# Reading the last five slots of a spilled transform back in halves: one FNet-style mixer with two feed-forward layers on one Trainium2 core

## The reference

```python
X = rfft(x, axis=1)
Yr = Xr @ w_r - Xi @ w_i + b_r
Yi = Xr @ w_i + Xi @ w_r + b_i
Y = soft_threshold(Yr, 0.01) + 1j * soft_threshold(Yi, 0.01)
y = irfft(Y, n=3008, axis=1)
# then on the 6016 tokens of y
h = y @ w_in;  y = (h * cos(h)) @ w_out          # 256 -> 2048 -> 256
h = y @ w_in2; y = (h * relu6(h + 3) / 6) @ w_out2
```

## Time and profile before

| | us |
|---|---|
| median of 3 runs | 1222.8 (1222.67 to 1222.94) |
| the profiled execution's own time | 1223.17 |
| its span, first to last instruction | 1221.4 |
| TensorE busy in it | 1201.1 (98%) |
| granted TensorE clock, mean | 0.994 of full speed |

### The profile page before, as it was taken

How to read it: one execution, slowest core, us unless ns; L and a number is a source line. 1 busy time by engine, 2 the same in 40 slices (tenths; PEclk the granted TensorE clock), 3 DMA queues, 4 the chain that set the end, 5 groups by cost and what they waited for, 6 DMA issues and landing times.

```text
span 1221.4 us, 14607 instructions
## 1 busy us (share of the span) xinstructions
PE 1201.1 (98%) x5576; PEld 1009.9 (83%) x5576; DVE 606.0 (50%) x599; ACT 631.1 (52%) x705; POOL 560.0 (46%) x294
## 2 busy tenths in 40 slices
PE   8999979899999999999999999999999999999998
PEld 8888779798888888888888888888888888888887
DVE  2787727655435445445454344444354354354344
ACT  2677646665545545445444445545455454454443
POOL 2577656774444433444334444344444444434410
PEclk9999989999999999999999999999999999999999
DMA  9488523000000100100001001001001001000000
GB/s 245 144 246 230 143 101 137 18 1 1 31 1 1 35 1 0 34 0 15 19 0 34 0 0 34 0 0 34 0 0 34 0 0 34 0 1 18 1 18 18
DMA packets 26149, 49.76 MB, mean 41 GB/s; under 512 B 3155, under 2 KB 9939, under 8 KB 25979
## 3 DMA queue, kind: packets, MB, share of 16 engines
q1 hardware_dynamic: 26114, 49.29, 13.4%
HBM read 31.06 MB, written 18.32 MB: 40 GB/s over the span
## 4 chain that ended last, share of the span: by engine, by line
PE 95%; DMA 2%; DVE 2%; ACT 1%; SPq 0%; issue 0%; POOL 0%; DVEq 0%; ACTq 0%
PE banks L586 41%; PE banks L636 41%; PE banks L491 2%; PE banks L511 2%; PE banks L506 2%; PE banks L507 2%; PE banks L564 2%; PE banks L526 1%; PE banks L527 1%; DMA v<-y_spill 1%; DMA y_spill<-y 1%; DMA xb<-in_x 0%; PE banks L542 0%; PE banks L540 0%; PE banks L539 0%; DVE phase L988 0%
## 5 line engine op out<-in xcount | busy, mean ns | idle before, releaser
L1167 POOL TENSOR_TENSOR gal<-ga,gah 128x1024 fp32r<-128x1024 f32 (+1 forms) x93 | 221.6, 2383 | 515.4 <-ACT gah L819 515.4
L984 DVE SCALAR_TENSOR_TENSOR phase<-phase,banks 128x1024 f32<-128x1024 int32 (+1 forms) x96 | 114.9, 1197 | 273.5 <-ACT phase L803 273.5
L1173 POOL TENSOR_TENSOR gbl<-gb,gbh 128x1024 fp32r<-128x1024 f32 (+1 forms) x88 | 206.6, 2348 | 16.6 <-ACT gbh L863 16.6
L811 ACT ACTIVATE cosine<-phase,half_pi 128x1024 f32<-128x1024 f32 (+1 forms) x96 | 109.1, 1136 | 192.8 <-DVE phase L988 192.1
L803 ACT ACTIVATE phase<-banks 128x1024 int32<-128x1024 f32 (+1 forms) x96 | 97.0, 1011 | 155.5 <-PE banks L586 154.9
L1006 DVE TENSOR_TENSOR ga<-banks,cosine 128x1024 f32<-128x1024 f32 (+1 forms) x96 | 115.4, 1203 | 104.8 <-ACT cosine L811 97.2
L1059 DVE SCALAR_TENSOR_TENSOR gb<-ramp,banks 128x1024 f32<-128x1024 f32 (+1 forms) x95 | 113.8, 1198 | 101.8 <-ACT ramp L848 101.8
L848 ACT ACTIVATE ramp<-banks,three 128x1024 f32<-128x1024 f32 (+1 forms) x95 | 104.3, 1098 | 108.9 <-PE banks L586 108.9
L863 ACT ACTIVATE gbh<-gb 128x1024 fp32r<-128x1024 f32 (+1 forms) x95 | 99.2, 1044 | 35.9 <-DVE gb L1059 31.6
L586 PE MATMUL banks<-xl,w1h 128*128 128x512 f32 (+1 forms) x384 | 116.8, 386 | 0.0
L586 PE MATMUL banks<-xh,w_lo 128*128 128x512 f32 (+1 forms) x384 | 116.7, 385 | 0.0
(11 more groups left out here) (107 smaller groups left out, 1853.1 us busy)
## 6 DMA issues: line engine op xcount, KB each, us to landing
w<-in_w_ff SPq DMA_DIRECT2D x32, 256.0 KB, 6.1
xb<-in_x SPq DMA_DIRECT2D x32, 192.0 KB, 6.7
y_spill<-y SPq DMA_DIRECT2D x24, 256.0 KB, 2.5
xf<-x_spill SPq DMA_DIRECT2D x11, 512.0 KB, 4.4
v<-y_spill SPq DMA_DIRECT2D x7, 780.0 KB, 7.1
x_spill<-xs SPq DMA_DIRECT2D x11, 470.0 KB, 3.2
out_y<-yt SPq DMA_DIRECT2D x10, 512.0 KB, 3.4
dbs<-in_db SPq DMA_DIRECT2D x24, 128.0 KB, 3.1
```

What stands on the lines that cost most here:

```text
L811: act.activation(cosine[:, :, 0:w], phase[:, :, 0:w], ACT.Sin, bias=half_pi[:, :], scale=-1.0).then_inc(a_cos, 1)
L984: dve.scalar_tensor_tensor(out=phase[:, :, 0:w], in0=phase[:, :, 0:w].bitcast(i32), scalar=-2.0 * math.pi, in1=bank[:, at:at + 2, 0:w], op ...
L1167: pool.tensor_tensor(gal[p % 2][:, :, 0:w], ga[:, :, 0:w], gah[p % 2][:, :, 0:w].bitcast(fp32), ALU.subtract).then_inc(a_gl, 1)
L1173: pool.tensor_tensor(gbl[pb % 2][:, :, 0:w], gb[:, :, 0:w], gbh[pb % 2][:, :, 0:w].bitcast(fp32), ALU.subtract).then_inc(b_gl, 1)
```

## The change

On SyncE, the seventh read of three whole slots (18 to 20) becomes three reads: the sine blocks (15 rows of 26 KB) at the old place, the cosine blocks (15 rows of 24 KB) later, and the cosine remainder (15 rows of 2 KB) behind write 23. Slots 21 and 22 are no longer read slot by slot in their sine blocks but together, as ten rows of 26 KB, after both are written. Their cosine remainder moves behind the read of slot 23 and is read with that slot's, 15 rows. The two remainder reads have a semaphore of their own, `v_rest_in`, which TensorE waits for before `cosine_part(12)`; before `cosine_part(0)` it now waits for three reads instead of four. The bytes read are the same.

```diff
-        v_idle_in = sem("v_idle_in")
+        v_idle_in, v_rest_in = sem("v_idle_in"), sem("v_rest_in")
...
             written(LAST_K - 3)
-            read_v(LAST_K - 2 - BATCHED, BATCHED, 0, BLOCKS, v_in)
+            read_v(LAST_K - 5, 3, FULL, FULL + 1, v_sin_in)
             for i in range(LAST_K - 2, LAST_K):
                 write_v(i)
             for i in range(LAST_K - 2, LAST_K):
                 written(i)
-                read_v(i, 1, FULL, FULL + 1, v_sin_in)
+            read_v(LAST_K - 2, 2, FULL, FULL + 1, v_sin_in)
+            read_v(LAST_K - 5, 3, 0, FULL, v_cos_in)
             read_v(LAST_K - 2, 2, 0, FULL, v_cos_in)
             write_v(LAST_K)
-            read_v(LAST_K - 2, 2, BLOCKS - 1, 1, v_cos_in)
+            read_v(LAST_K - 5, 3, BLOCKS - 1, 1, v_rest_in)
             written(LAST_K)
             read_v(LAST_K, 1, 0, FULL, v_cos_in)
-            read_v(LAST_K, 1, BLOCKS - 1, 1, v_cos_in)
+            read_v(LAST_K - 2, 3, BLOCKS - 1, 1, v_rest_in)
...
-            pe.wait_ge(v_in, 16 * (LAST_K - 2) // BATCHED)
+            pe.wait_ge(v_in, 16 * (LAST_K - 5) // BATCHED)
             pe.wait_ge(v_sin_in, 2 * 16)
             pe.wait_ge(v_idle_in, 16)
...
-            pe.wait_ge(v_cos_in, 4 * 16)
+            pe.wait_ge(v_cos_in, 3 * 16)
             for g in range(GROUPS):
+                if g == FULL:
+                    pe.wait_ge(v_rest_in, 2 * 16)
                 cosine_part(g)
```

## The result

The changed kernel takes 1220.24 us in the median of 16 runs (1219.63 to 1221.35), the kernel before 1222.84 (1222.22 to 1223.72): 2.60 us less, ratio 0.9979 with a 95% interval of 0.9971 to 0.9987. The forecast was 1220.0. The profiled execution has 1220.21 us with a span of 1218.4, so 1.8 us lie around the span, as before. The kernel before was run again beside each set of experiments; its median moved between 1222.47 and 1223.50 us from set to set, so medians of different sets are compared only through it.

A forecast was written before the change was run, and what follows sets the result against it. The prediction took TensorE's waits of 5.98 us at sine(0) and 0.50 us at cosine_part(0) as what could be gained. Its terms, 2.61 + 0.2 = 2.8 us, gave 1220.0 us, with a range of 1219.2 to 1221.8.

The forecast's parts named there:

- What bounds the kernel: TensorE's two waits on reads of v: 5.98 us at sine(0), 0.50 us at cosine_part(0); everything later hangs on TensorE.
- Part 1: Writes before sine(0): write 22 lands 1.99 us after issue, so SyncE's next issue comes 1.22 us earlier.
- Part 2: Joined sine read of slots 21 and 22 lands in 4.58 us; sine(0) 2.61 us earlier together with Part 1.
- Part 3: idft2(23)'s wait for y_lo from GpSimd: ready at 156.02, needed near 158.8, covered by 2.8 us.
- Part 4: Moved cosine reads ahead of write 23: engines clear by 158.1, write issued at 159.9, covered by 1.8 us, no cost.
- Part 5: cosine_part(0) no longer waits for the 10 KB remainder read: gain 0.2 us, between nothing and 0.50.
- The sum: Whole kernel: 2.61 + 0.2 = 2.8 us gained, from 1222.8 to 1220.0 us.
- over 0.2%: Whole kernel's median: faster by more than 0.2%, 2.45 us, so below 1220.35 us; chance 0.60.
- Rival B: Transfers before sine(0) hold each other up: write 22 takes 2.5 us, sine packets reach 5.3 us; 1221.4; chance 0.16.
- Rival C: TensorE's clock returns no earlier in the run, so sine matmuls end last before cosine_part(0); 1221.1 us; chance 0.07.
- Rival D: Queued reads share the engines instead of standing in line: sine(0) at 159.1, 1223.2 us; chance 0.07.
- Rival E: The change does not reach the end because something later has its own clock: 1222.8 us; chance 0.04.

The follow-up runs named there:

- e3: Kernel before, with only the cosine remainders on their own semaphore, waited for before cosine_part(12); 1222.73 us, ratio to before 0.9999.
- e1: Kernel before, with only the sine reads of slots 21 and 22 joined into one of ten rows; 1222.27 us, ratio to before 0.9992.
- e2: Kernel before, with only the read of slots 18 to 20 split into halves, sine reads of 21 and 22 separate; 1221.76 us, ratio 0.9988.
- e11: Changed kernel, with the joined sine read of slots 21 and 22 undone into two reads; 1220.86 us, ratio to before 0.9988.
- e6: Changed kernel, with both remainder reads waited for before cosine_part(0) again; 1220.38 us, ratio to before 0.9975.
- e7: Changed kernel, with the joined sine read cut: the seven blocks needed first, then the other six; 1218.64 us, ratio to before 0.9960.
- e4: Changed kernel, with the cosine read of slots 18 to 20 issued ahead of the joined sine read; 1221.99 us, ratio to before 0.9993.
- e5: Changed kernel, with unread matmuls added in TensorE's pauses around dft2(23), 6 ahead and 16 behind; 1223.00 us, ratio to before 0.9995.
- e9: Changed kernel, with unread matmuls added around dft2(23): 6 of 512 columns ahead, 32 of 256 behind; 1219.90 us, ratio to before 0.9976.
- e12: The same kernel as e9, run once more; 1219.24 us, ratio to before 0.9974.

## Why the prediction was right, and where its parts were not

**What bounds the kernel.** Right: two waits, 5.98 and 0.50 us, and nothing later took the gain back. The stretch from cosine_part(0) to the end is 1052.4 and 1052.3 us.

**Part 1, the freed writes.** Right: write 22 in 2.00 us (1.99 forecast). From write 21's issue to the first sine read 3.08 us instead of 4.25, 1.17 less (1.22 forecast).

**Part 2, the joined read.** Its landing was well priced (4.70 us, 4.58 forecast), and so was sine(0): 2.44 us nearer to write 21, 2.61 forecast. But of the "2.61 us for parts 1 and 2" part 1 had 1.22, which leaves 1.39 for the joining, and that split is wrong. sine(0) after write 21, in us, with two traces where there are two:

| | sine reads slot by slot | joined |
|---|---|---|
| slots 18 to 20 whole | 10.46, 10.02 (before, e3) | 9.88 (e1) |
| slots 18 to 20 in halves | 8.65, 8.47 (e2, e11) | 8.02, 8.17 (changed, e6) |

By the means the split is worth 1.7 to 1.8 us either way and the joining 0.4 to 0.5; both together 2.1 by these pairs, 2.44 by the first two traces alone. Four fifths of the gain are the first edit's. The pieces say why. Before, slot 22's read leaves 5.00 us after write 21: write 21 takes 4.23, and then SyncE spends 0.71 on slot 21's read first. In e11 it leaves after 3.02, as slot 21's read went out a microsecond before, so the split alone takes away SyncE's 0.7 us too, which the prediction had given to the joining. The read then takes 5.21 us to land in both, and the joining, which leaves at 3.08, only cuts that to 4.70. Why it is still 5.21 in e11, where its packets hardly wait for slot 21's, stays open. The sum came out right because it was taken along the chain and not as two gains; that it came within 0.2 us is in part luck, since single traces differ by 0.4.

**Part 3**, y_lo: covered, as said; sine(0) was followed by idft2 without a pause. **Part 4**: right, the engines were clear by 158.3 (158.1 forecast), write 23 left at 159.85 (159.9) and landed in 1.99 us.

**Part 5**, the remainders: 0.2 us forecast; 4.16 us from issue to landing against 4.39. e3 and e6 bound it between nothing and 0.3. In the four traces that wait for the remainders (before, e1, e2, e6) the data are there 3.9 to 4.4 us after the read's issue, in the changed kernel, e3, e11 and e7, which do not, after 3.8 to 4.3. The term is too small to be shown here, and nothing is as good a price as 0.2.

**The sum.** 2.8 us forecast; 2.67 to cosine_part(0) and 2.60 in the median. It lies beyond the 2.45 us of the 0.2% bound, but the interval (0.9971 to 0.9987) reaches past 0.998, so the "over 0.2%" that had 0.60 is not proved.

**Rival B**, slower transfers: no; 2.00 and 4.70 us. **Rival C**, the clock: this was closer than its 0.07. The fall itself moved: before the wait in the earlier trace rows, but only at 155 in the changed kernel. The return came 6.1 us after sine(0), and the sine matmuls ended 0.06 us ahead of the data. In e6 it came 3.1 us after and left 1.43 us, in e4 6.4 us after, and there the sine matmuls ended last. The Trainium skill's sentence that the chip judges on a free-running schedule (TensorE: Matmul & The Clock Gate, Part 1) agrees with such a spread between executions of nearly the same code. **Rival D**: out by e4. **Rival E**: out.

## What to carry to other kernels

When a long transfer sits in front of a short one that everybody waits for, cut the long one to what is needed by that time, and ask the same of the short one again: the second cut, e7, gained another 2.0 us from write 21 to the end beside the change's own 2.7, half of it by the clock. Price edits to one chain together, piece by piece along the chain; a right total says nothing about its parts, and here one part was priced three times too high and the other too low. Do each edit alone and undo each alone to see which one carried it, and take two traces of each where the parts are near the spread. And before a median is asked to show 0.1%, look for two events around the edit whose distance to the fixed parts of the kernel does not vary.

## What the runs showed of the hardware

A DMA that everybody waits for can take twice as long beside an instruction load: with 16 KB in one packet of 1.80 us on one engine write 23 landed in 4.23 us instead of 2.0 (e5), and with that packet moved ahead of the write, by 16 more matmuls, in 2.06 and 2.13 (e9, e12). The Trainium skill has the rule behind it (DMA: Bandwidth & Descriptors, Queues, rings and completion order: each engine serves its queues in turn, packet by packet); the trace agrees, as nine rows of e5 start only after the instruction packet, and this case adds what one such turn costs.

TensorE's return to 2.4 GHz came 5.8 us after sine(0) started in the kernel before, 6.1 in the changed one, 6.4 in e4 and 3.1 in e6, so a stretch of 48 sine matmuls took 6.81 us in the first and 5.53 in the last.

Outside the place of the change, these traces differ most in their first 47 to 49 us: the first write of y_spill was issued between 46.89 and 49.14 us after the start of the span. What makes that part vary stays open.
